# A recurrence and two routed layers on one core: second-part weights in slices, a new order of the routing, a two-operation leaky value

## The reference, cut to what matters

```python
def _attn_ref(q, k, v, i_gate, f_gate, o_gate):      # (4, 8, 768, 40)
    for t in range(S):                                # a gated recurrence per batch and head
        m_new = np.maximum(f_gate[t] + m, i_gate[t])
        f_stab = np.exp(f_gate[t] + m - m_new); i_stab = np.exp(i_gate[t] - m_new)
        C = f_stab * C + i_stab * outer(v[t], k[t]);  n = f_stab * n + i_stab * k[t]
        y[t] = sigmoid(o_gate[t]) * (C @ q[t]) / max(|n . q[t]|, 1)

def _moe_ref(x, w_gate, w1, w2):                      # x (3072, 320), 8 experts, w1 (320, 1024), w2 (1024, 320)
    # all (token, expert) pairs in order of falling logit; a token goes to the first expert that
    # still has room, room is 3072 / 8 = 384 tokens
    for e in range(E):
        out[mask] = np.maximum(x[mask] @ w1[e], 0.0) @ w2[e]

def _moe2_ref(x, w_in, w_out, alpha):                 # w_in (320, 2048), w_out (2048, 320)
    h = x @ w_in
    g = np.maximum(h, 0.0) + alpha * np.minimum(h, 0.0)   # the leaky value
    return g @ w_out
```

## Time and profile before

| | |
|---|---|
| median of 3 runs | 1102.79 us (1101.78 to 1103.4) |
| the profiled execution's own time | 1093.76 us |
| its span, first to last instruction | 1092.0 us |
| mean granted clock of TensorE | 0.863 of full |
| PE / DVE / ACT / POOL busy | 84% / 51% / 35% / 26% |

### The profile page before, as it was taken

How to read it: one execution, slowest core, us unless ns; L and a number is a source line. 1 busy time by engine, 2 the same in 40 slices (tenths; PEclk the granted TensorE clock), 3 DMA queues, 4 the chain that set the end, 5 groups by cost and what they waited for, 6 DMA issues and landing times.

```text
span 1092.0 us, 20456 instructions
## 1 busy us (share of the span) xinstructions
PE 919.2 (84%) x7118; PEld 855.8 (78%) x7118; DVE 551.5 (51%) x1521; ACT 381.1 (35%) x860; POOL 286.4 (26%) x295
## 2 busy tenths in 40 slices
PE   2779998989941898998798899889889989987996
PEld 2678888888831787888798788889788878987996
DVE  6524333443464356546555655654555565465343
ACT  5214222332202134424513432451352344235253
POOL 5304433445102301600610240051034016005201
PEclk9866656667755798999899999999989989999998
DMA  9964333333004003102100400300040031022000
GB/s 221 273 136 103 82 74 74 91 89 81 22 16 128 10 2 116 40 1 89 50 18 0 132 23 0 115 22 18 13 124 18 0 115 40 0 70 67 19 2 19
DMA packets 101171, 68.61 MB, mean 63 GB/s; under 512 B 67792, under 2 KB 91856, under 8 KB 100752
## 3 DMA queue, kind: packets, MB, share of 16 engines
q1 hardware_dynamic: 88368, 50.82, 17.6%
q10 hardware_dynamic: 10080, 8.65, 2.5%
q0 software_dynamic: 2688, 8.65, 2.5%
HBM read 59.46 MB, written 8.65 MB: 62 GB/s over the span
## 4 chain that ended last, share of the span: by engine, by line
PE 59%; DVE 12%; ACT 8%; issue 7%; POOL 5%; SPq 4%; DMA 1%; ACTq 1%; POOLq 1%; DVEq 0%
PE bank L747 13%; PE bank L749 11%; PE bank L748 11%; PE bank L656 6%; PE bank L693 5%; DVE g_act L1228 4%; DVE by_row L1183 3%; PE bank L761 2%; ACT h_hi L942 2%; PE bank L762 2%; PE bank L648 2%; PE bank L633 2%; ACT bank L940 2%; ACT g_neg L938 2%; SPq L377 2%
## 5 line engine op out<-in xcount | busy, mean ns | idle before, releaser
L523 POOL TENSOR_TENSOR w_lo<-s,w_hi 128x1024 fp32r<-128x1024 f32 x16 | 37.6, 2355 | 497.5 <-ACT w_hi L914 497.5
L1228 DVE SCALAR_TENSOR_TENSOR g_act<-g_neg,neg_alpha,bank 128x384 f32<-128x384 f32 x128 | 78.4, 613 | 102.4 <-ACT bank L940 101.5
L747 PE MATMUL bank<-wo_hi,h_hi 128*128 128x320 f32 x384 | 129.1, 336 | 0.3 <-DVE h_lo L1231 0.2
L749 PE MATMUL bank<-wo_hi,h_lo 128*128 128x320 f32 x384 | 122.7, 320 | 0.0
L748 PE MATMUL bank<-wo_lo,h_hi 128*128 128x320 f32 x384 | 122.4, 319 | 0.0
L1231 DVE TENSOR_TENSOR h_lo<-g_act,h_hi 128x384 fp32r<-128x384 f32 x128 | 80.5, 629 | 74.1 <-ACT h_hi L942 74.1
L942 ACT CAST h_hi<-g_act 128x384 fp32r<-128x384 f32 x128 | 65.6, 513 | 120.5 <-DVE g_act L1228 120.5
L938 ACT ACTIVATE g_neg<-bank 128x384 f32<-128x384 f32 x128 | 62.5, 488 | 108.4 <-PE bank L762 108.3
L936 ACT ACTIVATE h_hi<-bank 128x384 fp32r<-128x384 f32 x64 | 31.5, 492 | 188.4 <-PE bank L762 188.4
L747 PE MATMUL bank<-yT_hi,wi_hi 128*128 128x384 f32 x256 | 92.1, 360 | 0.1
L748 PE MATMUL bank<-yT_lo,wi_hi 128*128 128x384 f32 x256 | 90.1, 352 | 0.0
(11 more groups left out here) (197 smaller groups left out, 2079.3 us busy)
## 6 DMA issues: line engine op xcount, KB each, us to landing
s<-w SPq DMA_DIRECT2D x8, 1280.0 KB, 9.2
s<-w SPq DMA_DIRECT2D x8, 1024.0 KB, 5.2
s<-w SPq DMA_DIRECT2D x24, 256.0 KB, 6.3
sig<-o ACTq DMA_DIRECT2D x6, 640.0 KB, 9.2
q_in<-qT SPq DMA_DIRECT2D x48, 80.0 KB
q_wide<-qT SPq DMA_DIRECT2D x48, 80.0 KB
k_in<-kT SPq DMA_DIRECT2D x48, 80.0 KB
k_row<-k SPq DMA_DIRECT2D x48, 80.0 KB
```

The source lines that it names most:

```text
L523: pool.tensor_tensor(w1_lo[:, t, :], s1[:, t, :], w1_hi[:, t, :].bitcast(F32), ALU.subtract).then_inc(wlo_ready, 1)
L747: pe.matmul(acc, ah, bh, start=start, stop=False, skip_group_check=True)
L749: return pe.matmul(acc, al, bh, start=False, stop=stop, skip_group_check=True)
L1228: dve.scalar_tensor_tensor(out=g_act[:, n, :], in0=g_neg[:, n, :], scalar=neg_alpha[:, j:j + 1], in1=acc, op0=ALU.mult, op1=ALU.add).then_ ...
```

## The change

Second-part weights: SP loads them in sixteen slices of four transfers, each behind the load of tiles 4 to 19, and `high_piece` waits for its own slice. GpSimd's `weigh_values` is one tile ahead of `low_piece`. Routing beside an expert: `flag_full`, `raise_base` and `count_taken` stand earlier or later by a block, `close` stands ahead of `split_hidden`, its part for the next phase (`reopen`) is moved to j = 9, `match_rows` is one operation per third, `turn_rows` stands behind `down2`, `fetch_rows` behind the first `low_in`. The leaky value is acc + (1 - alpha) * relu(-acc): L940 goes.

```diff
-            def load_raw():
+            def load_raw(c, b):
+                i = B * (c - 1) + b
+                fs = bass.ds(PW * i, PW)
+                sp.wait_ge(prep_hi, 2 * i + 2)
+                sp.dma_start(wi_raw[:, :, fs], w_in[0:2 * P, fs].rearrange("(t p) f -> p t f", p=P)).then_inc(raw_in[b], 16)
+                sp.dma_start(rest_raw[0:REST, fs], w_in[2 * P:DM, fs]).then_inc(raw_in[b], 16)
+                sp.dma_start(rest_raw[REST:P, fs], w_in[2 * P:DM, fs]).then_inc(raw_in[b], 16)
+                sp.dma_start(wo_raw[:, bass.ds(i, 1), :], w_out[bass.ds(P * i, P), :].rearrange("(j p) d -> p j d", p=P)).then_inc(raw_in[b], 16)
...
-            load_raw()
-            with sp.Fori(1, NCH) as c:
+            with sp.Fori(1, NCH - 1) as c:
                 for b in range(B):
                     load_tile(c, b)
+                    load_raw(c, b)
+            for b in range(B):
+                load_tile(NCH - 1, b)
...
+            weigh_values(1, 0)
             with pool.Fori(1, NCH - 1) as c:
                 for b in range(B):
-                    weigh_values(c, b)
-                    low_piece(c, b)
+                    weigh_values(*nxt(c, b))
+                    low_piece(B * (c - 1) + b, b % 2)
...
             def get_expert(e):
                 low_in(e, 0)
+                fetch_rows(e)
                 low_in(e, 1)
-                fetch_rows(e)
-                low_out(e, 0)
                 low_in(e, 2)
-                low_out(e, 1)
-                low_out(e, 2)
+                for t in range(3):
+                    low_out(e, t)
...
                 up(J1, wi_hi, wi_lo, 0, yT_hi, yT_lo, y_ready, 3 * e)
+                if route:
+                    raise_base(ph, J1 - 1)
                 up(J1 + 1, wi_hi, wi_lo, 1, yT_hi, yT_lo)
...
-                    if route and j < 3:
+                    if route and 1 <= j < 3:
                         raise_base(ph, J1 + j - 1)
-                    if route and j == 3:
-                        count_taken(ph)
...
-                    if more and 11 <= j < 14:
-                        turn_rows(e + 1, j - 11)
                     down2(j)
                     if route and j < 2:
                         count(ph, J1 + j)
+                    if route and j == 2:
+                        count_taken(ph)
+                    if more and 11 <= j < 14:
+                        turn_rows(e + 1, j - 11)
...
+                act.wait_ge(raw_in[b], 64 * c)
                 act.copy(wo_hi[:, bass.ds(i, 1), :], wo_raw[:, bass.ds(i, 1), :]).then_inc(prep_hi, 1)
...
-                    act.activation(g_neg[:, k % 3, :], acc, ACT.Relu, scale=-1.0).then_inc(neg_ready, 1)
-                    act.wait_ge(neg_ready, J2 * e + k - J1 + 1)
-                    act.activation(acc, acc, ACT.Relu).then_inc(act_ready, 1)
+                    act.activation(g_neg[:, k % 3, :], acc, ACT.Relu, scale=-1.0).then_inc(act_ready, 1)
...
+            def reopen(ch):
+                ch.mark(dve.tensor_tensor(opened[:, :], need[:, :], cnt_sb[:, :], ALU.is_gt))
+                ch.link(dve.tensor_tensor(left[:, :], need[:, :], cnt_sb[:, :], ALU.subtract))
+                ch.mark(dve.scalar_tensor_tensor(out=need[:, :], in0=closed[:, :], scalar=FULL, in1=left[:, :], op0=ALU.mult, op1=ALU.add))
+                ch.link(dve.tensor_tensor(route_value[:, :, :], route_value[:, :, :], e_first(opened[:, :]), ALU.mult))
...
-                for c in range(8 * third, 8 * third + 8):
-                    ins = dve.tensor_scalar(by_row[:, c, :], count_bf[:, :], place_row[:, c:c + 1], None, ALU.is_equal)
-                ins.then_inc(onehot_ready, 1)
+                cs = slice(8 * third, 8 * third + 8)
+                dve.tensor_tensor(by_row[:, cs, :], count_bf[:, :].unsqueeze(1).to_broadcast([P, 8, P]), bc(place_row[:, cs], P),
+                                  ALU.is_equal).then_inc(onehot_ready, 1)
...
+                if route:
+                    flag_full(ch, ph, J1 - 1)
                 split_hidden(e, J1)
+                if route:
+                    compare(ch, ph, J1)
                 split_hidden(e, J1 + 1)
                 for j in range(J2):
+                    if route and j == 1:
+                        compare(ch, ph, J1 + 1)
                     if route and j == 2:
                         take(ch, ph)
                     if route and j == 3:
                         close(ch, ph)
+                    if j + 2 < J2:
+                        split_hidden(e, J1 + j + 2)
+                    if route and j < 2:
+                        flag_full(ch, ph, J1 + j)
```

More of the change, by code:

```diff
@@ L300, in build_program @@
         stage2_in = sem("stage2_in")
-        raw_in = sem("raw_in")
+        raw_in = [sem(f"raw_in{b}") for b in range(B)]
         prep_hi = sem("prep_hi")
@@ L486, in weigh_values, with low_piece @@
                                    ALU.mult).then_inc(faded, 1)
-            def low_piece(c, b):
-                i = B * (c - 1) + b
+            def low_piece(i, odd):
                 fs = bass.ds(PW * i, PW)
-                pool.wait_ge(prep_hi, 2 * i + 1)
+                pool.wait_ge(prep_hi, 2 * i + 9)
                 pool.sem_inc(waited, 1)
@@ L495, in low_piece @@
                                    ALU.subtract).then_inc(prep_lo, 1)
-                pool.wait_ge(prep_hi, 2 * i + 2)
+                pool.wait_ge(prep_hi, 2 * i + 10)
                 pool.sem_inc(waited, 1)
@@ L510, in _ @@
                 weigh_values(0, b)
+            weigh_values(1, 0)
             with pool.Fori(1, NCH - 1) as c:
                 for b in range(B):
-                    weigh_values(c, b)
-                    low_piece(c, b)
-            for b in range(B):
+                    weigh_values(*nxt(c, b))
+                    low_piece(B * (c - 1) + b, b % 2)
+            for b in range(1, B):
                 weigh_values(NCH - 1, b)
@@ L526, in low_in @@
                     pool.sem_inc(waited, 1)
-                    pool.wait_ge(wlo_ready, 6 * e + 3)
+                    pool.wait_ge(wlo_ready, 6 * e + 2)
                     pool.sem_inc(waited, 1)
@@ L765, in first_up @@
             def first_up(e):
-                pe.wait_ge(wlo_ready, 6 * e + 4)
+                pe.wait_ge(wlo_ready, 6 * e + 3)
                 up(0, w1_hi, w1_lo, 0, xT_hi, xT_lo, xe_ready, 3 * e)
@@ L896, in high_piece @@
                 act.copy(wi_hi[0:REST, 2, fs], rest_raw[0:REST, fs]).then_inc(prep_hi, 1)
+            act.sem_inc(prep_hi, 8)
             decays(0, 0)
@@ L900, in _ @@
                 step(0, b)
-            act.wait_ge(raw_in, 64)
             with act.Fori(1, NCH - 1) as c:
@@ L1208, in _ @@
             read_tokens(ch, 0)
+            reopen(ch)
             best(ch)
@@ L1226, in split_hidden @@
                     j = k - J1
-                    dve.scalar_tensor_tensor(out=g_act[:, n, :], in0=g_neg[:, n, :], scalar=neg_alpha[:, j:j + 1],
+                    dve.scalar_tensor_tensor(out=g_act[:, n, :], in0=g_neg[:, n, :], scalar=rest_alpha[:, j:j + 1],
                                              in1=acc, op0=ALU.mult, op1=ALU.add).then_inc(leaky_ready, 1)
@@ L1235, in expert @@
                 ch = chain_of(ph) if route else None
-                def search(n):
-                    if n:
-                        flag_full(ch, ph, n - 1)
-                    if n == len(VALUE_STEPS):
-                        keys_at_value(ch, ph)
-                    if n < NS:
-                        compare(ch, ph, n)
                 for k in range(1, J1):
                     if route:
-                        search(k - 1)
+                        if k > 1:
+                            flag_full(ch, ph, k - 2)
+                        if k - 1 == len(VALUE_STEPS):
+                            keys_at_value(ch, ph)
+                        compare(ch, ph, k - 1)
                     split_hidden(e, k)
                 if route:
-                    search(J1 - 1)
+                    flag_full(ch, ph, J1 - 2)
+                    compare(ch, ph, J1 - 1)
                 for t in range(3):
@@ L1254, in expert @@
                     dve.tensor_tensor(yT_lo[:, t, :], ACC[t][:, 0:CAP], yT_hi[:, t, :].bitcast(F32), ALU.subtract).then_inc(y_ready, 1)
+                if route:
+                    flag_full(ch, ph, J1 - 1)
                 split_hidden(e, J1)
+                if route:
+                    compare(ch, ph, J1)
                 split_hidden(e, J1 + 1)
                 for j in range(J2):
-                    if route and j < 3:
-                        search(J1 + j)
-                    if j + 2 < J2:
-                        split_hidden(e, J1 + j + 2)
+                    if route and j == 1:
+                        compare(ch, ph, J1 + 1)
                     if route and j == 2:
@@ L1272, in expert @@
                     if route and j == 9:
+                        reopen(ch)
+                    if route and j == 10:
                         best(ch)
```

30 lines of the change are left out of this document (12 added, 18 removed).

## The result

The changed kernel takes a median of 993.1 us (989.93 to 994.56, four runs) against 1102.28 us for the kernel before on the same chip: a ratio of 0.9007, interval 0.8982 to 0.9032. I had said 984 us, 945 to 1035.

A forecast was written before the change was run, and what follows sets the result against it. TensorE sets the pace everywhere, so its holes and lower-clock time can be won. Terms 16 + 38 + 62 + 3 = 119 off the profiled 1093.8 give 975, plus 9 for the median: 984 us, range 945 to 1035.

The forecast's parts named there:

- The stall, -16: Ahead of tile 4: slicing the raw weights removes a 13.1 us wait and the low-clock step behind it, -16 us.
- The recurrence's steps, 9.5 us: Recurrence, 20 steps: values one tile ahead end the `vw` waits; 190 us against 227.8, -38 us.
- the third rival: Recurrence: upper clock level holds and SP's 8.0 us sets the step; -68 in place of -38, 954 us; chance 0.17.
- The first rival: Recurrence keeps its clock pattern, steps lock to 10.3 us; -22 in place of -38, 1000 us; chance 0.20.
- The experts, -62: Seven routed experts: waits -54.6, clock -17, collisions +10, together -62 us.
- 0.3 remain: Wait at L741 for turning rows in each expert: 2.0 plus 0.5 us falls to 0.3.
- the +10 for collisions: Experts: VectorE operations running into GpSimd's cost +10 us, bounds 0 to 35.
- the 17 forecast: Experts: less time at the lower clock level, about one drop per expert remaining, -17 us.
- The second rival: Experts' holes move: blocked `h_lo` and shifted `split_hidden` give back half the gain, 31 us; 1015 us; chance 0.10.
- The leaky value, 0: Dropping L940 from ScalarE, 0.475 us per block, gives 0 by itself; it pays only in the L741 wait.
- Ahead of expert 0, -3: Before expert 0: earlier fetch -2.3 us, earlier `order` and shorter compares -0.7, together -3 us.
- The compare: Routing beside an expert: one operation per third takes 1.2 us; two SBUF inputs leave it exposed to GpSimd blocking (3.49 us before).

The follow-up runs named there:

- e3: The kernel before with the recurrence's changes alone (raw weights in slices, values one tile ahead): 1026.13 us, ratio 0.9336.
- e6: The kernel before with GpSimd's values one tile ahead alone, raw weights still loaded in one piece: 1021.5 us, ratio 0.9334.
- e7: The changed kernel with raw weights loaded for two tiles at once, behind every second tile (32 transfers instead of 64): 976.93 us, ratio 0.8889.
- e10: The changed kernel with e9's earlier `reopen` and `best` and e7's raw weights for two tiles at once: 924.91 us, ratio 0.8385.
- e9: The changed kernel with `reopen` behind `read_tokens` at j = 8 and `best` at j = 9: 945.87 us, ratio 0.8580.
- e12: The kernel before with the new order of routing and turning alone; old compare, fetch and leaky value: 1107.54 us, ratio 1.0059.
- e4: The kernel before with all changes except the recurrence's (routing, fetch, compare, leaky value): 1064.01 us, ratio 0.9688.
- e11: e9 with the old compare, 24 operations in place of three: 1009.84 us, ratio 0.9198.

## Why the prediction was right and where it was wrong

**The stall, -16.** Right: 16.1 us in e3. But it bought nothing beside the values ahead (e6 equals e3), since SP's longer list, which I had said has a cost, took it back. In the profiled execution after, the first tiles ran at the lower level and hid it. Why they start at one level in some executions and at the other in others is not settled.

**The recurrence's steps, 9.5 us.** The mechanism was right, the term mis-sized: 8.1 in the profile after and 8.6 in e3, so -55 to -66 in place of -38. I leaned on the one row of 10.10 us as if it were the pace without waits; it was a step partly at the lower level behind the stall. e6 shows that without `vw`'s wait the clock is up for most of the time, so the third rival (upper level, SP sets the pace) describes it better than the forecast. The third rival too was short in one thing: SP's list is 8.7 us and not 8.0, and PE outruns it for some tiles and then pays for a wait with the clock. That SP "cannot hold a step of the upper clock level for long" was right, and I found no price for it in rows; e7 and e10 give one, 13 and 21 us. The first rival was not empty: e6's three steps with the clock down and no wait took 10.1 to 11.6 us, near its 10.3. And what the prediction read out for the third, that work without long idle stretches stays at the full rate, did not hold there.

**The experts, -62.** The failed step is "0.3 remain" for the turn of rows, with the +10 for collisions set against it: 6.5 us remained in each expert. The other terms held: L703 kept 0.3 us an expert (0.8 forecast), L708 and L714 nothing, L725 0.8 (1.2 forecast). The clock gave 13.8 of the 17 forecast, if the excess is read as the clock's price. I named the mechanism, but looked for it in `h_lo` and the new compare (in e9, with the same compare and `h_lo` held more, neither made PE wait), and never priced that `reopen` at j = 9 pushes `best` to j = 10. The trace before had the operations of `best` at 358 ns on average, free, and I read that as their price anywhere. From the 2.3 us of waits that I had left in an expert to the 7.7 that stand there are 38 us in seven, a little past my upper bound of 35 for collisions. The second rival (half the experts' gain given back, 1015 us) is what the experts did, by another operation than it named. With `best` in e9's place the experts take 78 us less than before (734.9 to 656.9, first turn to the end), more than the 62.

**The leaky value, 0.** Wrong: 23 us by itself on the kernel before. "Nobody waits for `h_lo`" held for PE. It did not hold for VectorE's list, which I had as "counted above" in one wait only. Beside the other edits its share can't be told: it was not taken out of the changed kernel.

**Ahead of expert 0, -3.** 3.0.

**The compare.** Its price was right, 1.22 us, and its worth mis-read. I counted the difference of durations; it lies in not being held and in not delaying `best` into the subtractions. I also had it "not free of the 3.49". It does meet the subtraction in its last third, but as one operation that began first it was not held and held the subtraction instead. A place where it would begin behind a subtraction is not in these runs. The old form, which rows 7 show held, has one tensor and a column of scalars as its inputs, so it was no example of the two-input case that I set beside it.

The orderings together: the new order alone loses (e12), with the compare, the fetch and the leaky value it gains 34 us (e4), and with `reopen` and `best` one block earlier each, some 47 us more (0.9007 to 0.8580). An order by hand is worth what the durations are for which it is right.

## What to carry to other kernels

Before moving instructions on one engine, lay its list beside the other engine's that can hold it: here an operation of 0.36 us became 2.2 because it slid by one block into GpSimd's subtractions, and putting it back gave another 4.3% of the time before, where the whole change had given 9.9. An operation that no one waits for on TensorE can still set when all that stands behind it in its own engine's list comes out, so a chain's length is to be priced by who is queued, not only by PE's waits. And a queue of transfers has a length of its own: 13 transfers a tile, of 32 to 160 KB, took 8.7 us of it, and halving the number of the four added ones gave 13 to 21 us.

## What the runs showed of the hardware that was not expected

- A wait of 1.0 to 1.3 us in most steps of the recurrence went with a mean granted clock of 0.65 to 0.67; without it PE worked 75 us on end at 1.00 (e6). Then the clock fell to a mean of 0.57 for 28 us with PE busy all the time. A step with a wait can be longer by three times the wait: the one with 2.07 us took 13.16 us against 6.78.
- GpSimd's subtraction held the old compare in the middle: eight short operations that take 1.39 us together took 3.49 where a subtraction began 0.6 us behind their start (2.59 on average in e11). The same work as one operation, met by the subtraction at the same point, took its 1.22 us, and the subtraction took 2.86 instead of 2.34.
- Issuing a transfer in SP's loop took 0.30 to 0.87 us by itself, and not by its bytes: `q_wide` of 80 KB took 0.79 to 0.87, `wo_raw` of 160 KB 0.40 to 0.42, `rest_raw` of 32 KB 0.52 to 0.57.
- The granted clock in the windows of the changed kernel reads 1.00 from 28 to 52 us, where the matmuls' durations (0.47 us each for L624 against 0.24) show the lower level; the durations decide there.
